# Recurrent attention in chunks of 64 tokens instead of 128, with tokens loaded six to a partition

## The reference, cut to what matters

```python
# attention, for each of 2 x 8 heads, 768 tokens, head dimension 48
for t in range(S):
    cur = einsum('bhd,bhe->bhde', u * k[t], v[t])
    y[t] = einsum('bhd,bhde->bhe', r[t], state + cur)
    state = w[t][..., None] * state + einsum('bhd,bhe->bhde', k[t], v[t])
# then, on x = y laid out as (2, 768, 384):
h = gelu(x @ w_in); u, v = halves of h; v = layernorm(v) * g_ln
x = x + (u * (w_sg @ v + b_sg)) @ w_out
xk, xr = mixes of x with its previous token
out = sigmoid(xr @ w_r) * (relu(xk @ w_k) ** 2 @ w_v)
```

## Time and profile before

| | |
|---|---|
| median of 3 runs | 428.04 us (426.94 to 430.57) |
| span of the profiled execution | 429.3 us (time outside of the span is not shown) |
| PE busy | 399.1 us, 93% |
| DVE busy | 333.9 us, 78% |
| ACT busy | 207.5 us, 48% |
| POOL busy | 187.7 us, 44% |
| chain that ended last | PE 61%, DVE 27%, issue 8%, POOL 2% |

### The profile page before, as it was taken

How to read it: one execution, slowest core, us unless ns; L and a number is a source line. 1 busy time by engine, 2 the same in 40 slices (tenths; PEclk the granted TensorE clock), 3 DMA queues, 4 the chain that set the end, 5 groups by cost and what they waited for, 6 DMA issues and landing times.

```text
span 429.3 us, 7003 instructions
## 1 busy us (share of the span) xinstructions
PE 399.1 (93%) x2692; PEld 370.1 (86%) x2692; DVE 333.9 (78%) x484; ACT 207.5 (48%) x390; POOL 187.7 (44%) x184
## 2 busy tenths in 40 slices
PE   4699888979887898999999999999999999999997
PEld 3598877777767677887999899999999999999996
DVE  5999899999999999765555336797896993676951
ACT  4526765783758253468512315824793710465100
POOL 8779659948984888620000000250780000373000
PEclk9989999999999998999999999999999999999999
DMA  9999921890211011001200000402300002000011
GB/s 147 206 226 236 219 35 22 117 133 9 55 33 24 2 29 30 1 2 29 64 2 0 0 2 1 148 0 91 112 2 0 2 0 93 20 2 0 2 55 55
DMA packets 58305, 23.65 MB, mean 55 GB/s; under 512 B 52256, under 2 KB 55840, under 8 KB 58272
## 3 DMA queue, kind: packets, MB, share of 16 engines
q1 hardware_dynamic: 58272, 23.21, 25.9%
HBM read 18.49 MB, written 2.36 MB: 49 GB/s over the span
## 4 chain that ended last, share of the span: by engine, by line
PE 61%; DVE 27%; issue 8%; POOL 2%; DMA 1%; SPq 1%; ACT 0%; DVEq 0%; POOLq 0%
PE ps L1183 18%; PE ps L1184 18%; PE ps L1185 18%; DVE aT L901 11%; DVE kT L884 6%; PE ps L1172 3%; DVE bonus_rk L863 2%; DVE bonus_rk L858 2%; DVE r L888 2%; PE ps L1153 1%; POOL r L558 1%; PE ps L1150 1%; DVE a L871 1%; DMA ubc<-in_u_dram 1%; DVE sc L920 1%
## 5 line engine op out<-in xcount | busy, mean ns | idle before, releaser
L1172 PE MATMUL ps<-r,kT 112*128 112x128 f32 x672 | 90.9, 287 | 20.2 <-DVE aT L901 17.5
L1172 PEld LDWEIGHTS ps<-r,kT 112*128 112x128 f32 x672 | 82.9, 197 | 28.1 <-issue 25.7
L558 POOL TENSOR_TENSOR r<-r,wb 112x768 f32<-112x768 f32 x40 | 68.7, 1717 | 25.8 <-PE ps L1172 25.6
L901 DVE COPY_PREDICATED aT<-mask,ps 128x384 f32<-128x384 int8 x112 | 71.7, 705 | 0.0
L608 POOL TENSOR_TENSOR sq_f<-sq_f 128x384 f32<-128x384 f32 x32 | 33.8, 1071 | 74.9 <-ACT sq_f L757 74.8
L884 DVE TENSOR_TENSOR kT<-kT,wb 112x384 f32<-112x384 f32 x48 | 51.4, 1072 | 1.7 <-PE ps L1172 1.7
L603 POOL TENSOR_TENSOR wk_l<-wk_raw,wk_h 128x1024 fp32r<-128x1024 f32 x3 | 8.2, 2775 | 68.7 <-ACT wk_h L826 68.7
L1026 DVE TENSOR_TENSOR sq_l<-sq_f,sq_h 128x384 fp32r<-128x384 f32 x32 | 27.6, 864 | 10.4 <-ACT sq_h L762 10.4
L1185 PE MATMUL ps<-xk_h,wk_l 128*128 128x384 f32 x96 | 32.2, 335 | 0.0
L1184 PE MATMUL ps<-xk_l,wk_h 128*128 128x384 f32 x96 | 32.2, 335 | 0.0
L1183 PE MATMUL ps<-xk_h,wk_h 128*128 128x384 f32 x96 | 32.2, 335 | 0.0
(11 more groups left out here) (142 smaller groups left out, 973.0 us busy)
## 6 DMA issues: line engine op xcount, KB each, us to landing
tok_k<-in_k_dram SPq DMA_DIRECT2D x16, 144.0 KB, 4.6
tok_r<-in_r_dram SPq DMA_DIRECT2D x16, 144.0 KB, 5.0
tok_w<-in_w_dram SPq DMA_DIRECT2D x16, 144.0 KB, 4.3
sgn<-in_moe_w_sg_dram SPq DMA_DIRECT2D x6, 384.0 KB, 5.1
vt<-in_v_dram SPq DMA_DIRECT2D x16, 144.0 KB, 4.0
out_dram<-ot SPq DMA_DIRECT2D x12, 192.0 KB, 1.9
xT<-yT SPq DMA_DIRECT2D x12, 144.0 KB, 2.9
win_raw<-in_moe_w_in_dram SPq DMA_DIRECT2D x1, 1536.0 KB, 7.1
```

What stands on the lines that cost most here:

```text
L558: nc.gpsimd.tensor_tensor(t, t, pair_of(h, 0, q).unsqueeze(1).unsqueeze(3).broadcast_to([ROWS, 2, S // (2 * h), h]), ALU.mult).then_inc(r_ ...
L901: ins = nc.vector.copy_predicated(right2(aT[q % 4][:, :, g * HF:(g + 1) * HF], h), mask[:, l, :].rearrange("p (x n h) -> p x n h", x=2, h= ...
L1172: ins = nc.tensor.matmul(level[q % 2][:, c // 3, 0:HF].rearrange("p (x c t) -> p x c t", x=2, c=3)[:, :, c % 3, :], kT[q % 4][0:ROWS, c * ...
```

## The change

The chunk is 64 tokens, so there are 12 chunks and six levels, and a stage has 12 slots. Two neighbouring chunks share the partitions of aT: the first on 0 to 63, the second on 64 to 127, so aT has 6 x 2 x 64 elements a partition. A level job has 12 products, and from level 1 on their 384 score columns go to one bank, another bank for every second level. `take_level` is one masked copy.

The bonus moves into level 0. Level 0 uses copies of their own, kU and rU: r of even tokens and k of odd tokens are scaled by u there. The mask of level 0 includes the diagonal. `bonus`, `diagonals`, `join_r`, `lay_states` and `scale_last` go. `scale_r` is on DVE for levels 0 to 2 and on POOL for 3 to 5.

k, w and r are loaded as six consecutive tokens a partition, in rows of 1,152 bytes. The transposes become products with the identity, one for each head and group of tokens, and the ACT copies put the tokens in their natural order, so they write every sixth element. v is loaded as before. u comes as a column per pair. The side jobs, the pieces of the dense weights and the order of first loads are moved to other slots, and zeroing and masks are made anew at the start. The level job waits for the masked copy of two levels before instead of one.

Cut to its core:

```diff
+    CH = 64
+    NCH = S // CH
+    LEVELS = 6
...
+        plan = [[("kt", p0)], [("kt", p1)], [("u", p0), ("k", n0)], [("w", n0)], [("y", p0)], [("r", n0)],
+                [("u", p1), ("k", n1)], [("w", n1)], [("y", p1)], [("r", n1)], [], []]
...
+            plan[8:] = [[("y", p1), ("V", 0, 0)], [("V", 0, 1)], [("V", 0, 2)], [("V", 0, 3)]]
...
+            plan = [[("kt", p0), ("kt", p1), ("V", 0, 4)], [("u", p0), ("u", p1), ("V", 0, 5)], [("U", 0, 0)],
+                    [("U", 0, 1)], [("y", p0)], [("U", 0, 2), ("U", 0, 3)], [("y", p1)], [("U", 0, 4)],
+                    [("U", 0, 5)], [("U", 0, 6)], [("U", 0, 7)], []]
...
+    FIRST_TURNS = [("k", 0), ("w", 0), ("r", 0)]
...
+    DVE_R = 3
...
+              (1, 9): ("in", 4), (2, 1): ("in", 5), (2, 3): ("sg", 0), (2, 5): ("sg", 1),
+              (2, 7): ("sg", 2), (2, 9): ("sg", 3), (3, 1): ("sg", 4), (3, 3): ("sg", 5),
+              (3, 5): ("out", 0), (3, 7): ("out", 1), (3, 9): ("out", 2)}
...
+        aT = [up(f"aT{s}", [P, C, 2, CH], F32) for s in range(2)]
...
+                for kind, src in (("k", k), ("w", w), ("r", r)):
                     for x in range(2):
-                        sp.dma_start(tok[s][kind][:, :, 64 * x:64 * x + D],
-                                     src[b, 2 * p + x].rearrange("(c p) d -> p c d", p=P)
+                        sp.dma_start(tok[s][kind][:, x, 0:C * D], src[b, 2 * p + x].rearrange("(p c) d -> p (c d)", c=C)
...
+                        if l >= DVE_R:
...
+                        even, odd = [natural(rU[q % 2][lo:hi, x, :])[:, parity] for parity in range(2)]
+                        nc.scalar.activation(even, from_turn(src[lo:hi])[:, 0], ACT.Copy,
+                                             scale=ucol[lo:hi, q % PPB:q % PPB + 1])
+                        nc.scalar.copy(odd, from_turn(src[lo:hi])[:, 1])
+                    for x, (lo, hi) in enumerate(HEADS):
+                        ins = nc.scalar.copy(natural(r2[q % 4][lo:hi, x, :]), from_turn(src[lo:hi]))
...
+                    even, odd = [natural(kU[q % 2][0:ROWS, :])[:, parity] for parity in range(2)]
+                    nc.scalar.copy(even, from_turn(src[0:ROWS])[:, 0])
+                    nc.scalar.activation(odd, from_turn(src[0:ROWS])[:, 1], ACT.Copy,
+                                         scale=ucol[0:ROWS, q % PPB:q % PPB + 1])
+                    nc.scalar.copy(natural(kT[q % 4][0:ROWS, :]), from_turn(src[0:ROWS])).then_inc(copied, 1)
...
+            def scale_r(q, l):
+                h = 1 << l
                 if l == 0:
-                    t = right2(r2[q % 4][0:ROWS, :, :], 1)
-                    nc.vector.tensor_tensor(t, t, pair_of(1, 0, q).unsqueeze(1).unsqueeze(3)
-                                            .broadcast_to([ROWS, 2, S // 2, 1]), ALU.mult).then_inc(r_first, 1)
+                    dve.wait_ge(copied, turn_at[("r", q)] + 1)
+                else:
+                    dve.wait_ge(r_scaled_dve, r_by_dve(q, l - 1))
+                t = right2(r2[q % 4][0:ROWS, :, :], h)
+                nc.vector.tensor_tensor(
+                    t, t, pair_of(h, 0, q).unsqueeze(1).unsqueeze(3).broadcast_to([ROWS, 2, S // (2 * h), h]),
+                    ALU.mult).then_inc(r_scaled_dve, 1)
...
             def take_level(q, l):
                 h = 1 << l
+                dve.wait_ge(scores, level_at(q, l) + 1)
                 if l == 0:
-                    if q < 2:
-                        dve.wait_ge(first_diag[q], 1)
-                    else:
-                        dve.wait_ge(diag_made, 2 * C * (q - 1))
-                if q == 0 and l in (0, 2):
-                    dve.wait_ge(mask_made, 1 + l // 2)
-                for g in range(2):
+                    if q < 4:
+                        dve.wait_ge(zeroed, A_ZEROED[q])
+                    if q == 0:
+                        dve.wait_ge(mask_halved, 1)
                     ins = nc.vector.copy_predicated(
-                        right2(aT[q % 4][:, :, g * HF:(g + 1) * HF], h),
-                        mask[:, l, :].rearrange("p (x n h) -> p x n h", x=2, h=h),
-                        level[q % 2][:, g, 0:HF].rearrange("p (x n h) -> p x n h", x=2, h=h))
+                        aT[q % 4][:, :, :, :].rearrange("p (b c) x t -> p b (c x) t", b=2),
+                        mask_first[:, 0:CH].unsqueeze(1).unsqueeze(1).broadcast_to([P, 2, C, CH]),
+                        level[q % 2][:, :, 0:HF].rearrange("p b (m t) -> p b m t", t=CH))
+                else:
+                    dve.wait_ge(masked, level_at(q, l - 1) + 1)
+                    if q == 0:
+                        dve.wait_ge(mask_halved, 2)
+                    ins = nc.vector.copy_predicated(
+                        right(aT[q % 4][:, :, :, :].rearrange("p c x t -> p (c x t)"), h),
+                        mask[:, l - 1, 0:CH // 2].unsqueeze(1).broadcast_to([P, 2 * C, CH // 2])
+                        .rearrange("p m (n h) -> p m n h", h=h),
+                        level[q % 2][:, l % 2, 0:HF].rearrange("p (m n h) -> p m n h", m=2 * C, h=h))
...
+                for n in range(NCH - 1):
+                    new, inc = sc[q % 2][0:ROWS, n, 0:D], y_banks(q)[0:ROWS, n % 2, n // 2 * D:(n // 2 + 1) * D]
...
+                        if l < DVE_R:
+                            scale_r(q, l)
...
-                        ins = nc.tensor.transpose(dst[0:ROWS, c // 3, (c % 3) * P:(c % 3 + 1) * P],
-                                                  tok[q % 2][kind][:, c, 0:ROWS], ident[:, :])
+                        for x, (lo, hi) in enumerate(((0, 64), (64, ROWS))):
+                            ins = nc.tensor.matmul(dst[lo:hi, c % 2, c // 2 * P:(c // 2 + 1) * P],
+                                                   tok[q % 2][kind][:, x, c * D:c * D + hi - lo], ident[:, :],
+                                                   start=True, stop=True)
...
+            def u_job(q):
+                pe.wait_ge(copied, turn_at[("kt", q)] + 1)
+                pe.wait_ge(v_in[q % 4], 32 * (q // 4 + 1))
+                if 0 < q < NP - 1:
+                    pe.wait_ge(y_copied, q)
+                for c in range(C):
+                    for g in range(2):
+                        if 2 * c + g == NCH - 1:
+                            continue
+                        for lo, hi in ((0, 64), (64, ROWS)):
+                            ins = nc.tensor.matmul(y_banks(q)[lo:hi, g, c * D:(c + 1) * D], ktok[q % 2][CHUNK[g], c, lo:hi],
+                                                   vt[q % 4][CHUNK[g], c, lo:lo + D], start=True, stop=True)
+                ins.then_inc(increments, 1)
...
+            def y_job(q):
+                pe.wait_ge(states, (NCH - 1) * (q + 1))
                 pe.wait_ge(masked, level_at(q, LEVELS - 1) + 1)
-                pe.wait_ge(r_last, q + 1)
-                if q % 2:
-                    pe.wait_ge(y_copied, 2 * (q - 1) + part + 1)
-                for c in range(3 * part, 3 * (part + 1)):
-                    cols = slice(c % 3 * P, (c % 3 + 1) * P)
-                    if c:
-                        nc.tensor.matmul(ybank[part][0:ROWS, cols], st[q % 2][0:ROWS, c - 1, 0:ROWS],
-                                         rU[q % 2][0:ROWS, c * P:(c + 1) * P], start=True, stop=False)
-                    for x, (lo, hi) in enumerate(HEADS):
-                        ins = nc.tensor.matmul(ybank[part][lo:hi, cols], vt[q % 4][:, c, lo:hi],
-                                               aT[q % 4][:, x, c * P:(c + 1) * P], start=(c == 0), stop=True)
+                pe.wait_ge(r_scaled_pool, r_by_pool(q, LEVELS - 1))
+                y = y_banks(q)
+                for n in range(1, NCH):
+                    for x, (lo, hi) in enumerate(((0, 64), (64, ROWS))):
+                        nc.tensor.matmul(y[lo:hi, n % 2, n // 2 * CH:(n // 2 + 1) * CH], sc[q % 2][0:ROWS, n - 1, 0:hi - lo],
+                                         r2[q % 4][0:ROWS, x, n * CH:(n + 1) * CH], start=(n < 3), stop=False,
+                                         skip_group_check=True)
+                for n in range(NCH):
+                    for x, (lo, hi) in enumerate(((0, 64), (64, ROWS))):
+                        ins = nc.tensor.matmul(y[lo:hi, n % 2, n // 2 * CH:(n // 2 + 1) * CH], vt[q % 4][CHUNK[n % 2], n // 2, lo:hi],
+                                               aT[q % 4][CHUNK[n % 2], n // 2, x, :], start=False, stop=True,
+                                               skip_group_check=True)
...
+                    if l <= DVE_R:
+                        pe.wait_ge(r_scaled_dve, r_by_dve(q, l - 1))
                     else:
-                        pe.wait_ge(r_scaled, r_scaled_at(q, l - 1))
-                    pe.wait_ge(masked, level_at(q, l - 1) + 1)
+                        pe.wait_ge(r_scaled_pool, r_by_pool(q, l - 1))
+                    pe.wait_ge(masked, level_at(q, max(l - 2, 0)) + 1)
                 for c in range(C):
-                    ins = nc.tensor.matmul(
```

(69 more changed lines are left out.)

358 lines of the change are left out of this document (124 added, 234 removed).

## The result

The changed kernel takes **472.3 us** (median of 4 runs, 471.5 to 478.6) against 427.8 in the same session (4 runs, 426.9 to 430.6): a ratio of 1.102, 95% interval [1.097, 1.107]. I had said 411. A ratio leaves out runs more than 1.5% above the fastest of the same kernel, here the one of 478.6. The profiled execution took 472.59 us, its span is 470.7 and its granted clock 0.906 (before: 429.3 and 0.992).

The account below looks back on a forecast made before the run. DVE, without slack and sharing one queue of two-operand work with POOL, was taken as the bound. Stages 1 to 3 -14.9, start +1, stage 4 -3: -16.9 from 428.04 gives 411 us; forecast 400 to 418, range 393 to 428.

Parts of the forecast that it names:

- I take x1: ACT's copies writing every sixth word: no slowdown from the stride, 768 elements in 0.79 us; bounds x1 and x1.8.
- Rival 3: ACT's strided copies take twice as long: +11 before level 0 of pair 1, +3 for each of three waits; 430, chance 0.10.
- PE stands 1.2 us at k(n1): PE at slot 6 waits 1.2 us for banks held by r's ACT copies from slot 5; POOL's low half hides it.
- rival 2: PE and the turn banks become the bound: a stage of 38 gives 418, another half-rate dip 424; chance 0.14.
- The sign that the prediction gave for being wrong: DVE standing idle waiting for PE for more than 4 us a stage.
- The x0.92 rule: Stages 1 to 3: a stage takes 0.92 of summed DVE two-operand and POOL work, plus 1 us: 35.2, 36.5, 39.8.
- rival 5: PE's column halves do not pair for these shapes: 47 us of PE a stage, 445; chance 0.04.
- Turns as products: PE turns of 24 records take 1.4 us instead of 0.7, +4 a stage, hidden by the DVE and POOL queue.
- Stage 0: Start and first attention stage: 54 us against 53.1, counted +1, bounds -5 and +5.
- Dense rest: Last stretch after the attention stages, PE full and no line changed: carried over at about 222 us.
- Stages 3 and 4: Last full attention stage and the one draining it: 39.8 and 25, 64.8 us together.
- The sum of queues: DVE's two-operand work and POOL's work counted as one queue in stages 1 to 3: 14.9 us saved, bounds 18 and 9.

Follow-up runs that it names:

- early release: On the changed kernel with PSUM read in token order, ACT copies plain r and k out first, freeing the turn banks; u-scaled halves come later from SBUF: 425.1 us.

## Why the prediction was wrong, step by step

**"I take x1"** on ACT's strided copies is the step that failed. The rows had no such write, and of two DVE rows with a stride of two words I passed over the one that I had called the nearest, the masked copy with x1.8, and took the scaling (0.59 against 0.55), for a stride of six words on another engine. It is x1.9 to 2.0 (793 to 1,507 ns). Dense writes alone give 36 of the 44 us back. It is not the only step: with the factor of one in place the kernel takes 436 to 438 us, still outside of the range of 393 to 428, for the wait at the turn banks below. The copies with half the elements were too cheap as well: 0.43 us was the estimate, 0.46 and 0.58 is what dense ones take.

**Rival 3** had this very factor and priced it +20. The changed kernel is at +61 from the forecast: the mechanism was right and its price a third. I counted +11 at the start, where slot 1 is over 5.9 us later than forecast, and three waits of k(n1) at +3, near what each wait grew by itself (4.9 instead of 1.2). Missing were, in stage 0 alone, the turns of w_sg, which use the same banks (5.68, 3.22 and 5.67 us of PE waits in 57 to 82 us), and k, w, r of two more pairs; and PE at its lower clock behind each wait. Slot 1 was over at 39.4 instead of 33.5, and slots 2 to 11 took 45.7 instead of 20.6 us.

**"PE stands 1.2 us at k(n1)", hidden by POOL's low half.** It stands 4.9 (110.79 and 157.53), and nothing hides it: DVE and POOL wait for the level jobs that queue behind. Even with dense copies the wait (2.1 us) is not covered; early release takes it away and wins 12.7 us in all. So rival 2 (turn banks as the bound, 418 to 424) was right about the mechanism, and too cheap: with the factor of one it is 436 to 438. Its 418 does not follow from its stage of 38 either: three of those are 114 us, 2.5 more than the 111.5 of the forecast, which makes 414. The sign that the prediction gave for being wrong, DVE idle for PE for more than 4 us a stage, came: 70.2 us ahead of its scalings of k.

**DVE and POOL.** Their work was right. Masked copies take 26.5 (L810, x40) and 8.2 us (L802, x8), 34.7 in all against 32 predicted; the scaling of k has a mean of 742 ns ("near 0.8"); POOL works 22 to 26 us a stage. The x0.92 rule gave 35.2 and 36.5, and the early-release kernel takes 34.75 and 37.78; there the engines' busy times leave 4.5 us of PE and 5.6 of DVE idle in the first of these stages, so the agreement may be luck in part.

**PE.** Level jobs take 0.87 to 0.92 us ("about 1.0"), turns 1.5 ("1.4"): the column halves pair, rival 5 is dead. Turns as products, which I had "hidden", cost 13 us with the strided copies, as they lie in the loop; with the short loop they cost nothing that the runs can tell (425.1 and 424.5).

**Stage 0**, +1 predicted, is +32; with the loop short it is +1.7 (54.78). **Dense rest**: 221.5, as predicted.

**Stages 3 and 4**: -8 predicted, about 0 in the changed kernel and +0.7 with early release. The sum of queues holds no order. Levels 0 to 2 need DVE alone, so POOL's joins and low halves collapse onto DVE's first slots (5.33 us); the last four slots are PE's (a level job and a dense group, 3.1 us a slot, 3.4 before), whatever DVE saves. The first is shown: its removal made the stage 3.2 us shorter, of which 1.9 were lost behind it. That the second holds the rest is read from the timeline and was not tested.

**The miss, added up.** The profiled span is 58.3 us above the forecast's (429.3 - 16.9 = 412.4): stage 0 31.1, stage 1 9.1, stage 2 10.8, stages 3 and 4 7.7, dense rest -0.3. Of the early-release kernel it is 9.7 us above, and 8.8 of these lie in stages 3 and 4; that part of the forecast fails even with the copies and the banks put right.

## What to carry to other kernels

Before pricing an engine's work, follow who frees the buffer it works from: a copy that nobody counts as busy is on the path when the next product needs its bank, and every user of that bank pays. Free a shared PSUM buffer with the fewest copies and make derived tiles from SBUF afterwards (12.7 us here, and 28 where the derived tiles also lost their wide stride). Where ACT must reorder a layout on the way out of PSUM, try the jumps on the PSUM side first: here they cost nothing there and 35 us on the SBUF side.
